# Attention and two MLPs on one core: all batches' short pieces first, x kept on chip, scores in the MLP's banks

## The reference

```python
scores = scale * np.matmul(q, k.transpose(0, 1, 3, 2))
scores = np.where(causal, -1000000000.0, scores)
a = softmax(scores)                       # over the keys
local = np.matmul(a, v)
q_p = phi(q)                              # q + 1 above zero, exp(q) below
mem_out = (q_p @ M_prev) / (q_p @ z_prev + 1e-06)
attn = g * mem_out + (1 - g) * local      # g = sigmoid(beta), per head
x = attn.transpose(0, 2, 1, 3).reshape(2304, 512)
h = x @ w_in;  y = G(h) @ w_out           # G(h): h above 1, 0 below -1, (h + 1)^2 / 4 between
out = leaky(y @ w_in2) @ w_out2           # leaky(h) = max(0.01 h, h)
```

## Time and profile before

| | before |
|---|---|
| time, median of 3 runs | 1087.18 us (1084.54 to 1088.27) |
| the profiled execution | 1086.95 us |
| its span, first to last instruction | 1085.2 us |
| PE busy | 1036.4 us (96%), 7840 matmuls |
| ACT, POOL, DVE busy | 561.5, 470.8, 450.3 us |
| mean granted clock of PE | 0.975 of full |
| DMA | 72.82 MB, mean 67 GB/s |

### The profile page before, as it was taken

How to read it: one execution, slowest core, us unless ns; L and a number is a source line. 1 busy time by engine, 2 the same in 40 slices (tenths; PEclk the granted TensorE clock), 3 DMA queues, 4 the chain that set the end, 5 groups by cost and what they waited for, 6 DMA issues and landing times.

```text
span 1085.2 us, 19947 instructions
## 1 busy us (share of the span) xinstructions
PE 1036.4 (96%) x7840; PEld 971.6 (90%) x7840; DVE 450.3 (41%) x1109; ACT 561.5 (52%) x1280; POOL 470.8 (43%) x444
## 2 busy tenths in 40 slices
PE   4568999999999999999999999999999999999998
PEld 3457999999999999999999999999999999999997
DVE  6677765656565565656531126411111111111111
ACT  6767877676776777777743346422222222222221
POOL 3765855646475645556441238422222222222221
PEclk9667999999999999999999999999999999999999
DMA  5553222233232322233211045110101101011000
GB/s 168 152 154 114 62 77 85 75 92 85 72 94 77 90 80 62 81 88 93 72 58 40 1 147 184 59 39 1 40 1 39 40 1 39 1 39 40 1 20 20
DMA packets 89949, 72.82 MB, mean 67 GB/s; under 512 B 48000, under 2 KB 79360, under 8 KB 89856
## 3 DMA queue, kind: packets, MB, share of 16 engines
q1 hardware_dynamic: 89856, 71.55, 22.6%
HBM read 57.68 MB, written 13.78 MB: 66 GB/s over the span
## 4 chain that ended last, share of the span: by engine, by line
PE 89%; ACT 3%; DVE 2%; POOL 2%; issue 2%; DMA 1%; SPq 0%; POOLq 0%; DVEq 0%; ACTq 0%
PE Hp L402 13%; PE Hp L403 12%; PE Hp L404 12%; PE Yp L419 7%; PE Yp L420 6%; PE Yp L421 6%; PE Yp L425 6%; PE Yp L426 6%; PE Yp L427 6%; PE At L367 5%; PE At L356 5%; PE At L316 3%; PE At L339 1%; ACT prob L449 1%; DVE WBl L675 1%
## 5 line engine op out<-in xcount | busy, mean ns | idle before, releaser
L806 POOL TENSOR_TENSOR Gl<-Gl_raw,Gh 128x512 fp32r<-128x512 f32 x144 | 196.5, 1365 | 382.2 <-ACT Gh L564 382.1
L402 PE MATMUL Hp<-Xh,WAh 128*128 128x256 f32 x1152 | 331.1, 287 | 0.0
L403 PE MATMUL Hp<-Xl,WAh 128*128 128x256 f32 x1152 | 326.3, 283 | 0.0
L404 PE MATMUL Hp<-Xh,WAl 128*128 128x256 f32 x1152 | 326.3, 283 | 0.0
L402 PEld LDWEIGHTS Hp<-Xh,WAh 128*128 128x128 f32 x1152 | 220.8, 192 | 7.0 <-issue 2.5
L403 PEld LDWEIGHTS Hp<-Xl,WAh 128*128 128x128 f32 x1152 | 221.1, 192 | 2.7
L404 PEld LDWEIGHTS Hp<-Xh,WAl 128*128 128x128 f32 x1152 | 221.0, 192 | 0.0
L687 DVE TENSOR_TENSOR Gl_raw<-Hp,Gl_raw 128x512 f32<-128x512 f32 x72 | 49.8, 692 | 314.6 <-ACT Gl_raw L556 314.6
L419 PE MATMUL Yp<-Gh,WBh 128*128 128x256 f32 x576 | 169.8, 295 | 0.5 <-POOL Gl L806 0.5
L556 ACT ACTIVATE Gl_raw<-Hp 128x512 f32<-128x512 f32 x72 | 43.1, 598 | 243.7 <-PE Hp L404 243.7
L420 PE MATMUL Yp<-Gl,WBh 128*128 128x256 f32 x576 | 162.6, 282 | 0.0
(11 more groups left out here) (86 smaller groups left out, 1749.3 us busy)
## 6 DMA issues: line engine op xcount, KB each, us to landing
WAl_raw<-w_in SPq DMA_DIRECT2D x16, 512.0 KB, 4.8
WBl_raw<-w_out SPq DMA_DIRECT2D x16, 512.0 KB, 4.6
bc<-rn_scratch SPq DMA_DIRECT2D x32, 160.0 KB, 3.1
Vs_raw<-vv SPq DMA_DIRECT2D x16, 320.0 KB, 3.5
Kl_raw<-kk SPq DMA_DIRECT2D x16, 288.0 KB, 3.4
yT_scratch<-xraw SPq DMA_DIRECT2D x9, 512.0 KB, 3.8
xraw<-yT_scratch SPq DMA_DIRECT2D x9, 512.0 KB, 3.8
out<-xraw SPq DMA_DIRECT2D x9, 512.0 KB, 2.8
```

Of the source, the lines that this page charges most:

```text
L402: pe.matmul(h, WAh[:, f, j, :], Xh[:, c % 2, j, :], start=(j == 0), stop=False)
L403: pe.matmul(h, WAh[:, f, j, :], Xl[:, c % 2, j, :], start=False, stop=False)
L404: last = pe.matmul(h, WAl[:, f, j, :], Xh[:, c % 2, j, :], start=False, stop=(j == DT - 1))
L806: gp.tensor_tensor(Gl[:, U % 2, :], act[:, U % 2, :], Gh[:, U % 2, :].bitcast(F32), ALU.subtract).then_inc(g_lo, 1)
```

## The change

- `part(n)` and `pair(n)` put part 0 of all batches in slots 0 to 15 and part 1 in slots 16 to 31. G0 goes from 54 to 46, so the first MLP matmul is in tick 42: slot 5, k = 2.
- Chunks 0 to 3 are queries 0 to 255 of batches 0 to 3, chunks 4 to 7 are queries 256 to 511, and chunk 8 has the last 64 of each. Of a part-0 slot's 320 queries the first 256 go straight from xt to Xh and Xl by the new `split_slot(last)`, on ACT and DVE at k = 1 in every slot; the other 64 go to DRAM (`store_tail`) and come back in the part-1 slot of the same pair (`load_tail`), where they stand ahead of its 256. The last 64 of part 1 go to DRAM for chunk 8. `load_chunk` is left for chunk 8 and the second MLP, whose chunks are taken in the order `SECOND`.
- `scores` of slots 0 to 4 go to Hp and Yp.
- `qraw`, `kraw` and `phi` have memory of their own. `load_qk` waits for the low parts of the slot before instead of for its scores. `least_q` moves from k = 3 to 1, `q_high` from 5 to 2, `k_high` and `k_low` from 5 to 4.
- `memory_out` and `sums_out` move ahead of `exps(n, 1)` on ACT.
- `finish` moves from k = 1 to k = 0 on POOL; for slots 8 on, `scale_memory` is taken out of it and stands at k = 7 of the slot before. `mem` has two buffers, `bc` one.

The core of the diff:

```diff
 def part(n):
-    return n % 8 // 4
+    return n // PAIRS
 def pair(n):
-    return 4 * (n // 8) + n % 4
+    return n % PAIRS
...
-G0 = 54
+G0 = 46
...
+OTHER_BANKS = 5
+SECOND = [0, 1, 2, 3, 4, 5, 6, 8, 7]
...
+def splits(c):
+    return 4 * (c + 1) if c < CHUNKS - 1 else SLOTS + 2 * (c - CHUNKS + 2)
...
+        def score_bank(n, h):
+            bank = At[:, 2 * h:2 * h + 2, :] if n >= OTHER_BANKS else (Hp, Yp)[h][:, :, :]
+            return bank.rearrange("p a c -> p (a c)")
+        def x_place(n):
+            return slice(TAIL * part(n), QL[0])
...
             def load_qk(n):
-                after(sp, s_done, n)
+                after(sp, phi_done, n)
+                after(sp, q_lo, n)
+                after(sp, k_lo, n)
...
+            def store_tail(n):
                 sp.wait_ge(x_done, n + 1)
+                after(sp, tail_stored, 16 * n)
+                to = left_dram[pair(n)] if part(n) == 0 else last_dram[j, :, TAIL * i:TAIL * i + TAIL]
+                sp.dma_start(to, xt[:, C:C + TAIL]).then_inc(tail_stored, 16)
+            def load_tail(n):
+                sp.wait_ge(tail_stored, 16 * n)
+                sp.wait_ge(x_lo, n)
+                sp.dma_start(xt[:, 0:TAIL], left_dram[pair(n)]).then_inc(tail_in, 16)
...
             def scores(n):
                 pe.wait_ge(q_lo, n + 1)
                 pe.wait_ge(k_lo, n + 1)
-                after(pe, x_sum, 2 * (n - 1))
-                after(pe, pt_lo, 4 * (n - 1))
+                if n < OTHER_BANKS:
+                    after(pe, max_done, tiles_before(n))
+                else:
+                    pe.wait_ge(x_sum, 2 * (n - 1))
+                    pe.wait_ge(pt_lo, 4 * (n - 1))
+                    pe.wait_ge(mem_out, 2 * n)
...
             def hidden(U, a):
                 if U % UNITS == 0 and a == 0:
-                    pe.wait_ge(x_lo, 2 * c + 2)
+                    pe.wait_ge(x_lo, splits(c))
...
         ACT, slot(n, k):
-                if front is not None and k in (1, 2):
-                    exps(front, k - 1)
+                if front is not None and k == 1:
+                    exps(front, 0)
+                if k == 1 and last is not None:
+                    split_slot(last)
                 if k == 2 and front is not None:
                     memory_out(front)
                 if k == 2 and back is not None:
                     sums_out(back)
+                if k == 2 and front is not None:
+                    exps(front, 1)
+                if k == 2 and coming is not None:
+                    q_high(coming)
...
+            def split_slot(n):
+                c, j = n // 4, n % 4
+                sc.wait_ge(x_done, n + 1)
+                if part(n) == 1:
+                    sc.wait_ge(tail_in, 16 * (n - PAIRS + 1))
+                after(sc, h_done, 2 * UNITS * (c - 1))
+                sc.activation(Xh[:, c % 2, j, :], xt[:, 0:C], ACT.Copy).then_inc(x_hi, 1)
...
         DVE:
-                if k == 3 and coming is not None:
+                if k == 1 and coming is not None:
                     least_q(coming)
+                if k == 1 and last is not None:
+                    split_slot(last)
...
         POOL:
             def finish(n):
-                gp.wait_ge(bc_in, 32 * n + 32)
                 gp.wait_ge(x_sum, 2 * n + 2)
+                gp.tensor_tensor(x, x, bc[:, 0, 0:ql], ALU.mult).then_inc(x_scaled, 1)
+                gp.wait_ge(x_scaled, n + 1)
+                gp.tensor_tensor(x, x, bc[:, 1, 0:ql], ALU.add).then_inc(x_done, 1)
...
-                if k == 1 and last is not None:
-                    finish(last)
                 if k == 0 and back is not None:
                     v_low(back)
+                if k == 0 and last is not None:
+                    if last < UNITS:
+                        gp.wait_ge(v_lo, last + 2)
+                        scale_memory(last)
+                    finish(last)
...
+                if k == 7 and back is not None and back >= UNITS:
+                    scale_memory(back)
```

More of the change, by code:

```diff
@@ L240, in slot @@
                     load_qk(front + 1)
-                if k == 3 and last is not None:
-                    store_x(last)
+                if k == 2 and last is not None:
+                    store_tail(last)
                 if k == 2 and front is not None and front + 1 < SLOTS:
@@ L248, in slot @@
                     send_sums(back)
+                if k == 4 and back is not None and part(back) == 1:
+                    load_tail(back)
                 if k == 5 and back is not None:
@@ new lines, in store_chunk @@
+                    return
+                t = SECOND[c - CHUNKS]
+                if t < CHUNKS - 1:
+                    row = S * (t % 4) + C * (t // 4)
+                    sp.dma_start(out[row:row + C, :].rearrange("(a p) d -> p a d", p=P), yout).then_inc(out_stored, 16)
+                else:
+                    for b in range(B):
+                        row, r = S * b + 2 * C, TAIL * (b % 2)
+                        sp.dma_start(out[row:row + TAIL, :], yout[r:r + TAIL, b // 2, :]).then_inc(out_stored, 16)
@@ L315, in both_heads @@
                         r = slice(D * h, D * h + D)
-                        last = pe.matmul(At[0:rows, 2 * h + col // 512, col % 512:col % 512 + keys],
+                        last = pe.matmul(score_bank(n, h)[0:rows, col:col + keys],
                                          qt[r, q0:q0 + rows], kt[r, k0:k0 + keys], start=(step == 0), stop=(step == 2))
@@ L381, in slot @@
                     if front is not None:
-                        pe.wait_ge(max_done, tiles_before(front) + NT[part(front)])
+                        after(pe, pt_lo, 4 * (front - 1))
+                        if front >= OTHER_BANKS:
+                            pe.wait_ge(max_done, tiles_before(front) + NT[part(front)])
                     if back is not None:
@@ L462, in memory_out @@
                 sc.wait_ge(mem_done, n + 1)
-                after(sc, mem_scaled, 2 * (n - 2))
+                after(sc, mem_scaled, 2 * (n - 1))
                 for h in range(2):
-                    sc.activation(mem[:, n % 3, h, 0:ql], At[:, h, 0:ql], ACT.Copy).then_inc(mem_out, 1)
+                    sc.activation(mem[:, n % 2, h, 0:ql], At[:, h, 0:ql], ACT.Copy).then_inc(mem_out, 1)
             def weights_high(b, h):
@@ L497, in f_high @@
                 sc.wait_ge(phi_done, n + 1)
+                after(sc, mem_done, n)
                 sc.activation(Fh[:, 0:ql], phi[:, 0:ql], ACT.Copy).then_inc(f_hi, 1)
@@ L509, in slot @@
             def slot(n, k):
[L510 removed]
+                front, back, last = stage(n)
                 coming = n + 1 if n + 1 < SLOTS else None
[L512 to L513 removed]
+                if front is not None and k == 1:
+                    exps(front, 0)
+                if k == 1 and last is not None:
+                    split_slot(last)
                 if k == 2 and front is not None:
@@ L523, in slot @@
                     phi_exponent(coming)
-                if k == 5 and coming is not None:
-                    q_high(coming)
+                if k == 4 and coming is not None:
                     k_high(coming)
@@ L640, in least_q @@
                 ve.wait_ge(q_in, 16 * n + 16)
-                after(ve, mem_done, n)
+                after(ve, f_lo, n)
                 ve.tensor_scalar(phi[:, 0:ql], qraw[:, 0:ql], 0.0, None, ALU.min).then_inc(q_min, 1)
@@ L655, in slot @@
             def slot(n, k):
-                front, back, _ = stage(n)
+                front, back, last = stage(n)
                 coming = n + 1 if n + 1 < SLOTS else None
```

147 lines of the change are left out of this document (72 added, 75 removed).

## The result

The changed kernel takes 1102.97 us (median of 4 runs, 1102.23 to 1103.31) against 1086.62 for the kernel before on the same chip: a ratio of 1.0151 with a 95% interval of [1.0131, 1.0170]. It is slower, as forecast, and 7 us slower than the 1096 forecast. The profiled execution took 1103.31 for a span of 1101.5.

A forecast was written before the change was run, and what follows sets the result against it. It took attention alone to bound the head and PE the rest: span 1085.2 - 6.5 + 13.0 = 1091.7, plus 2.1 for chunk starts = 1093.8, plus 1.75 and 0.2 = 1095.8, say 1096; range 1080 to 1106.

The forecast's parts named there:

- X(2): Head, slot 2: POOL's `finish` first raises x_done at 36.5, about 1 us sooner than the path before would give.
- three head loops: Head, slots 2 to 5: x_done to x_done through ACT and POOL takes 16.5 each, giving X(5) = 86.0.
- slot 5 to 6: MLP's start: loop of 21.2 with two `hidden` ticks and transposes on PE first, then POOL's 10.3.
- 6 to 8, two slots: Slots 6 to 8: loop of 18.5 each against PE's 16.53, so PE stalls 2 us in each.
- Step (1): Slot order: attention left at chunk 1's start grows by 13.0 us; break-even only if chunk 1 starts before 154.
- Step (2): On-chip x hand-over: a loop through ACT and POOL delays the MLP to 87.0 and chunk 1 to 160.6; span 1091.7.
- f_low starts at X + 7.6: Head slot: x_done to POOL's f_low takes 7.6, including 1.1 for head 1's exps and q_high.
- Step (3): Later chunk starts: DVE's unit, `least_q` and split finish late, 0.3 + 4 x 0.45 = 2.1 us for chunks 2 to 6.
- Step (4): Score banks, two mem buffers, V's landing and last-chunk DMAs: priced at 0; V costs 0.6 a slot if landing takes 5.
- A: Head, no loop: slots go at 13.5, MLP starts at 73.5, chunk 1 at 137.5, time 1071.5; chance 0.15.
- B: Head, short loop of 15 a slot and later PE stalls vanish: chunk 1 about 147, time 1081; chance 0.08.
- C: Slots 6 and 7: PE's idle lowers its clock, some 7 us: 1103, to 1112 with chunk stalls; chance 0.12.

The follow-up runs named there:

- run 1: Changed kernel with ACT and DVE splitting x at position 5 instead of 1 in slots that complete no chunk, piece tails loaded later: 1103.69 us, ratio 1.0152.
- run 4: Changed kernel with the edits of run 1 and run 2 together: 1092.43 us, ratio 1.0050 to the kernel before.
- run 2: Changed kernel with POOL's two weight splits moved behind `finish`, to the next slot's start, from in front of `v_low`: 1088.68 us, ratio 1.0011.
- run 10: Kernel of run 9 with 7 extra unused matmuls in each of slots 1 to 4: 1086.06 us, ratio 0.9994 to the kernel before.
- run 9: Run 2 plus late x splits in slots 2 to 4, third mem buffer, DVE's x split before `phi_sum` there and before `least_q` elsewhere: 1085.78 us, ratio 0.9988.
- run 12: Run 2 plus late x splits in slots 2 to 4 only, and DVE's x split before `least_q` from slot 5 on: 1083.66 us, ratio 0.9974.
- run 7: Changed kernel with 14 extra unused matmuls in each of slots 1 to 4 to keep PE busy: 1098.25 us, ratio 1.0102 to the kernel before.
- run 3: Changed kernel with all scores going to At again instead of Hp and Yp in the first slots: 1102.22 us, ratio 1.0136 to the kernel before.
- run 8: Changed kernel with late x splits in the three head slots and a third mem buffer, POOL's order as it is: 1093.65 us, ratio 1.0057.

## Why the prediction was right, and where its sizes were off

The likeliest case is what happened: the loop from x_done to x_done exists, and the change is slower. The sum was 1093.8 against a span of 1101.5.

| term | forecast | measured | off |
|---|---|---|---|
| X(2), first x_done | 36.5 | 38.6 | +2.1 |
| three head loops | 49.5 | 53.0 | +3.5 |
| slot 5 to 6 | 21.2 | 22.9 | +1.7 |
| 6 to 8, two slots | 37.0 | 37.9 | +0.9 |
| 8 to 9, copies | 16.4 | 16.5 | +0.1 |
| order, later stalls | 13.0 + 2.1 | 14.45 | -0.65 |

All but the last term came out longer than forecast, so the sum owes little to errors that cancel.

*Step (1), order.* Right: every kernel with this order and this G0 whose positions are known has 931.9 to 932.6 left (but runs 1 and 4, whose late splits go with stalls at the chunk starts), 13.8 to 14.5 more than before, of which 13.7 is PE's busy time for my 13.0. Chunk 1 had to start before 154 to break even. The runs bear that line out as closely as they can be told apart: with chunk 1 at 156.0 the time is 0.11% longer (run 2), at 153.6 and 153.2 0.06% and 0.12% shorter (runs 10 and 9), at 148.5 0.26% shorter (run 12).

*Step (2), the hand-over.* Right in kind. All that I named is in the trace: Xh's idle before it of 3.7 in slots 2 to 4 (I said 3 to 4), slots of 18.9 at 6 and 7, no stall in steady slots. The size that failed is "so f_low starts at X + 7.6": it was 8.25. In it, "I take 1.1" for head 1's exps and q_high was too little. From `memory_out` to Fl the kernel before took 6.1 (50.39 to 56.49), the changed one 7.92 (38.93 to 46.85). The difference, 1.8, is all that exps and q_high take (1.4 + 0.4): in the changed kernel the first PTh follows q_high without a wait, and from there on the two paths are equally long (`values` starts 1.41 behind the first PTh in both). I had let 0.7 of it hide behind the transposes; nothing hid. The rest, 8.9 from Fl on, was 9.4: the weights' low parts and v_low took 3.43 + 1.0 where I took 3.0 + 1.0 from the shorter of two rows. Beside other work of DVE they took 2.98 + 1.44 (run 7), the same sum.

PE's rate is in this path, but was not the error. In my expectation of run 7 I blamed the half clock for 1.2 us of the miss; but `values` took 2.9 in the stretch from which I built the 6.1 too (ACT's and PE's timelines of the kernel before):
```profile
51.19 0.67 ACT L473 ACTIVATE PTh<-At 128x320 fp32r<-128x320 f32 x2
...
52.60 0.61 PE L367 MATMUL At<-PTh,Vs 128*128 128x320 f32 x1
53.00 0.47 PE L367 MATMUL At<-PTl,Vs 128*128 128x320 f32 x1
53.27 0.36 PE L367 MATMUL At<-PTh,Vs 128*128 128x192 f32 x1
```
The spacing is 0.27 here as well. What run 7 shows is what the full rate would give: Fl at X + 6.9. The rate was part of two other misses. X(2): Fl came 1.06 later than before (29.18 for 28.12) and POOL's path from there is 9.4 in both; `values` started no sooner (25.19 for 25.08), so the gain of 1 did not come, and took 2.9 for 2.0 at the full rate, which is the loss of 1. Slot 5 to 6: the second tick of `hidden` took 2.5 at the lower rate where I had 1.5 (1.0 of the 1.7), and POOL's part 10.9 for 10.3.

*Step (3), later chunk starts.* The mechanism was right: PE waits 0.79 for DVE's Xl at chunk 1, and putting the split before `least_q` gave 0.7 in all (runs 9 and 12). But at chunks 2 to 6 PE waits only 0.15 to 0.18 each, 0.84 in all, where I had priced 2.1; its idle time behind chunk 1 grew by 0.7 (5.9 for 5.2).

*Step (4), the rest at 0.* The banks: right (run 3). V's landing: right, no wait in the changed kernel; a shorter loop takes this cover away too, and then V holds the slot (runs 9 and 10). mem's two buffers: 0 only under the cover of the x_done wait, as I had reasoned; run 1 took the cover away and 1.9 us stood there. I hadn't said what it would cost then.

*Rivals.* A (no loop) is refuted by Xh's wait of 3.7, B (a short one) by the slot of 17.7. The head loop comes down to B's 15 and below only when ACT's waits are moved (13.8, 14.6 and 15.4 in run 8), and stays there with POOL's weights moved too (14.0, 13.9 and 14.2 in run 12). C, a low clock in slots 6 and 7, is refuted: the clock record has one stretch of 3.4 us at 0.5, at 112.3, and none later before chunk 1, and the matmuls of `hidden` take 0.28 each from 115.8 on, for 0.41 inside the stretch. The argument that I had against C was a misreading, though: of the 31.71 us from 95.94 on PE was busy 31.06, so they held 0.65 us of idle time and not 3 us of stalls; most of the 3 us was the lower clock (a mean of 0.94 over 31.7 us is 1.9). A's sum has a slip as well: 73.5 + 44.7 + 18 is 136.2, not 137.5.

What stays open is how the late splits of runs 1 and 4 reach the chunk starts, and how far the best head slot (run 12, 14 us) could still fall: there POOL waits 1.7 for ACT's Vs, and ACT 0.2 to 0.3 for V's load.

## What to carry to other kernels

When in-order engines hand work to each other once per stage, add the path from a wait's release back to itself through every queue it crosses, and compare it with the slot: here no engine was over 60% busy in a head slot and the loop alone set 17.7 us. Moving one wait can show only the next in line (x_done, then mem, then DVE's Xl, then V's load), whereas moving 3.4 us a slot of unrelated work from in front of the hand-over to behind it gave 13 us at once. Count an overlap as hidden only where a row shows the slack; the 0.7 us that I let hide behind the transposes came back in full. A pipeline reordered to start the second stage sooner also leaves more of the first for the stretch where the shared engine is full: write down the break-even start before you write the code.

## What the hardware showed that I hadn't expected

- The granted clock is printed as 1.00 for a head whose matmuls are spaced at 1.2 GHz, where no clock record exists before 98.7; other runs of the same family have records there (0.5 from 24.3 to 82.3 in run 12). The Trainium skill (TensorE: Matmul & The Clock Gate, Seeing it yourself) warns that clock records can be unreliable; by that rule, the trace agrees.
- Useless matmuls made a kernel faster: a ratio of 1.0102 for 1.0151, with 56 extra matmuls in the trace, since PE's rate doubled for part of the head (0.15 for 0.27 us between the same two matmuls).
- DVE and POOL slow each other. DVE's x split took 0.42 us alone and 1.47 beside POOL's weight split (run 9). POOL's pair of weight splits took 2.50 beside DVE's PTl, which has one input in SBUF (run 12), and longer beside DVE's own two weight splits: 3.43 in the changed kernel's head slots and 3.0 in slots 5 to 7, where the next POOL instruction took 1.45 for 1.00. The Trainium skill (SBUF — State Buffer, Who interferes with whom) says that a DVE instruction with two SBUF inputs contends with a GpSimd instruction that reads SBUF; the splits are of that form, and the trace agrees.
